# A gated scan with two feed-forward layers: first loads in halves on two queues, turns set among products, output weights loaded by rows

## The reference

```
f = lower_bound + (1 - lower_bound) * sigmoid(f_logit)
h[t] = f[t] * h[t-1] + (1 - f[t]) * x[t]              (per batch and channel)
z = relu(h @ w_in1) ** 2 @ w_out1
g = z @ w_in2 ;  out = where(g > 0, g, exp(min(g, 0)) - 1) @ w_out2
```

## Time and profile before

| | us |
|---|---|
| median of 3 runs | 1981.14 (1980.86 to 1981.81) |
| profiled execution, its own time | 1982.25 |
| its span | 1980.5 |
| PE busy | 1968.4 |
| DVE busy | 1575.6 |
| ACT busy | 1510.4 |
| POOL busy | 608.8 |

### The profile page before, as it was taken

One profiled execution on the slowest core, in us unless ns is written; L12 is line 12 of the kernel. 1 busy time (PEld: TensorE's weight loads), 2 busy tenths in 40 slices (PEclk: granted clock), 3 DMA queues, 4 the chain that ended last, 5 costly groups with the idle time before them and its releaser, 6 DMA issues.

```text
span 1980.5 us, 27947 instructions
## 1 busy us (share of the span) xinstructions
PE 1968.4 (99%) x8746; PEld 1638.7 (83%) x8746; DVE 1575.6 (80%) x1766; ACT 1510.4 (76%) x1818; POOL 608.8 (31%) x506
## 2 busy tenths in 40 slices
PE   8999999999999999999999999999999999999998
PEld 6887888888888888888888888888888888888888
DVE  5656888888888888888888888878888887866887
ACT  7887778778778777777877777777777787777766
POOL 3455323223232232332323323223232232322410
PEclk9999999999999999999999999999999999999999
DMA  5679444444444444344444444434444443443453
GB/s 168 198 210 266 152 139 121 147 146 132 131 137 137 123 146 146 115 146 137 126 135 146 135 134 135 138 107 156 146 125 143 137 124 116 147 128 121 139 171 111
DMA packets 244291, 283.09 MB, mean 143 GB/s; under 512 B 170433, under 2 KB 180674, under 8 KB 244162
## 3 DMA queue, kind: packets, MB, share of 16 engines
q1 hardware_dynamic: 241250, 280.23, 46.6%
q10 hardware_dynamic: 2912, 1.51, 0.3%
HBM read 249.30 MB, written 32.37 MB: 142 GB/s over the span
## 4 chain that ended last, share of the span: by engine, by line
PE 97%; ACT 1%; DMA 1%; issue 0%; SPq 0%; DVE 0%; ACTq 0%
PE acc L586 51%; PE ring L586 45%; DMA o_sb<-in_moe_w_in_dram 0%; PE acc L739 0%; DMA xa<-in_f_logit_dram 0%; PE ring L729 0%; ACT xa L985 0%; ACT xa L980 0%; ACT xb L980 0%; SPq L404 0%; ACT xb L985 0%; ACT hid_hi L1043 0%; ACT hid_hi L1053 0%; ACT wout L919 0%; DVE y_raw L1442 0%
## 5 line engine op out<-in xcount | busy, mean ns | idle before, releaser
L586 PE MATMUL acc<-hid_hi,wout 128*128 128x512 f32 (+1 forms) x3072 | 1142.4, 387 | 1.4 <-DVE wout L1277 1.3
L586 PE MATMUL ring<-t_hi,s_w 128*128 128x512 f32 (+1 forms) x2720 | 1035.7, 387 | 2.5 <-ACT m_sb L1064 1.4
L586 PEld LDWEIGHTS acc<-hid_hi,wout 128*128 128x128 f32 x3072 | 576.6, 188 | 115.7 <-DVE hid_lo L1361 2.2
L586 PEld LDWEIGHTS ring<-t_hi,s_w 128*128 128x128 f32 x2720 | 510.6, 188 | 104.9 <-ACT m_sb L1064 1.8
L586 PE MATMUL acc<-hid_lo,wout 128*128 128x512 f32 (+1 forms) x1536 | 594.7, 387 | 0.0
L586 PE MATMUL ring<-t_lo,s_w 128*128 128x512 f32 (+1 forms) x1360 | 526.6, 387 | 0.0
L1690 POOL TENSOR_TENSOR xb<-xb,m_sb 128x512 f32<-128x512 f32 (+1 forms) x176 | 225.9, 1284 | 965.4 <-DVE hid_lo L1361 960.8
L1064 ACT ACTIVATE m_sb<-ring 128x512 f32<-128x512 f32 (+1 forms) x176 | 104.6, 594 | 365.2 <-PE ring L586 345.7
L586 PEld LDWEIGHTS acc<-hid_lo,wout 128*128 128x128 f32 x1536 | 288.3, 188 | 56.5
L586 PEld LDWEIGHTS ring<-t_lo,s_w 128*128 128x128 f32 x1360 | 255.3, 188 | 50.6
L1361 DVE TENSOR_TENSOR hid_lo<-xa,hid_hi 128x1024 fp32r<-128x1024 f32 (+1 forms) x191 | 231.4, 1211 | 80.6 <-ACT hid_hi L1043 80.5
(11 more groups left out here) (117 smaller groups left out, 1711.9 us busy)
## 6 DMA issues: line engine op xcount, KB each, us to landing
s_w<-s_kept SPq DMA_DIRECT2D x184, 512.0 KB, 3.8
s_w<-s_kept SPq DMA_DIRECT2D x176, 384.0 KB, 4.1
wout<-w_kept SPq DMA_DIRECT2D x96, 512.0 KB, 4.4
out_dram<-o_sb SPq DMA_DIRECT2D x88, 128.0 KB, 3.5
f_raw<-in_f_logit_dram SPq DMA_DIRECT2D x168, 64.0 KB, 3.5
x_raw<-in_x_dram SPq DMA_DIRECT2D x168, 64.0 KB, 2.7
s_kept<-ee SPq DMA_DIRECT2D x16, 512.0 KB, 3.8
s_kept<-s_w SPq DMA_DIRECT2D x8, 512.0 KB, 3.9
```

The lines of the kernel that those rows point to most:

```text
L586: mm = nc.tensor.matmul(out_ap, lhs[a], rhs[b], start=start and t == 0, stop=stop and t == 2)
```

## The change

- `load_first` loads half of a 512 KB tile, 256 KB. The halves of f of batch 1 are the first issue on SP and on ACT, then come the halves of x of batch 1. f of batch 0 is also split over the two queues; x of batch 0 goes out as two halves on SP, behind the first two pairs' raw weights. The row of `lower_bound` moves from SP to ACT.
- `turn` takes one chunk. PE's order is f chunk 0, `lower_bound`, f chunk 1, x of batch 1, 4 matmuls on zeros in place of 16, f chunk 0 of batch 0; the other three turns stand between the first products.
- ACT makes the gates of batch 0 ahead of the cast of batch 1's second chunk, and `weights_hi_out(1, 0)` stands before the first relu. DVE's order follows.
- The second layer's output weights are loaded with one DMA of whole rows for a pair; ACT and DVE put the columns in order, with two instructions of 128x256 each in place of one of 128x512.
- In the phase of order 1, SP issues the next pair's raw loads before the stores, the quarters of f and x in steps 1, 4 and 5 at the end in place of 1, 4 and 6 near the start, and `load_s` before `load_sums`. `load_s` of the first pairs has a wait of its own.
- The last quarter's `tanh` of block 2 and the last pair's `weights_hi_out`/`weights_lo_out` of layer 2 move from the end of order 1 into step 0 of order 2, behind the copies of m1 and m2. `keep_w2` of that pair moves behind the first `load_w2`.

```diff
-WARM = (8, 16)
+WARM = (8, 4)
...
+        def load_first(eng, src, b, dst, loaded, half):
+            o = dst[:, b, half].rearrange("p (k d) -> p k d", d=D)
+            rows = src[b, half * HALF:(half + 1) * HALF, :].rearrange("(k p) d -> p k d", p=P)
+            eng.dma_start(o, rows).then_inc(loaded[b], DMA_INC)
...
+        def columns_in(t, c):
+            return t.rearrange("p j (a c e) -> p c j a e", c=CH, a=G)[:, c]
+        def columns_new(t, c):
+            return t[:, :, c * P:(c + 1) * P].rearrange("p j (a e) -> p j a e", a=G)
...
-        W_LOADS = {1: DMA_INC, 2: 2 * CH * DMA_INC}
+        W_LOADS = {1: DMA_INC, 2: DMA_INC}
...
     (load_raw_out, second layer)
-                for j in range(2):
-                    for c in range(CH):
-                        sp.dma_start(o[:, j, c * P:(c + 1) * P].rearrange("p (a e) -> p a e", e=SQ),
-                                     wout2_v[:, 2 * p + j, :, c, :]).then_inc(wr_loaded[0], DMA_INC)
+                sp.dma_start(o, wout2_v[:, 2 * p:2 * p + 2, :]).then_inc(wr_loaded[0], DMA_INC)
...
     (load_s)
-                if not (isinstance(pr.s, int) and pr.s < 2):
+                if isinstance(pr.s, int) and pr.s < 2:
+                    sp.wait_ge(up_n0, pr.g - 1)
+                else:
                     sp.wait_ge(m4_done, pr.s - 1)
...
+            QUARTER_AT = {1: 1, 4: 2, 5: 3}
...
     (SP's phase, order 1)
                         if p < PAIRS - 1:
                             load_q(ahead(p + 1))
                         else:
+                            load_s(ahead(p + 1))
                             load_sums(ahead(p + 1))
-                            load_s(ahead(p + 1))
-                        if p in (1, 4, 6):
-                            load_f(2, (p + 1) // 2)
-                            load_x(2, (p + 1) // 2)
+                        if 1 <= p < PAIRS - 1:
+                            load_raw_in(2, p + 1)
+                        load_raw_out(2, p)
                         if p >= 1:
                             keep_w2(p - 1)
-                        load_raw_out(2, p)
                         keep_q(2, p)
                         if p == 0:
                             keep_sums(1, PAIRS - 1)
                         else:
                             keep_sums(2, p - 1)
-                            if p < PAIRS - 1:
-                                load_raw_in(2, p + 1)
+                        if p in QUARTER_AT:
+                            load_f(2, QUARTER_AT[p])
+                            load_x(2, QUARTER_AT[p])
                         continue
                     if known(ph.order, 2) and p == 0:
+                        load_s(ahead(1))
                         load_sums(ahead(1))
-                        load_s(ahead(1))
                     if known(ph.order, 2) and p == 0:
                         keep_sums(2, PAIRS - 1)
-                        keep_w2(PAIRS - 1)
...
                     if ph.layer == 2:
                         sp.wait_ge(down_n0, g - 1)
                         load_w2(pair_of(ph, p))
-            load_first(sp, f_logit, 1, xa, f0_loaded)
-            sp.dma_start(lb_row, lower_bound.rearrange("(o d) -> o d", o=1)).then_inc(lb_loaded, DMA_INC)
+                    if known(ph.order, 2) and p == 0:
+                        keep_w2(PAIRS - 1)
+            load_first(sp, f_logit, 1, xa, f0_loaded, 0)
+            load_first(sp, x, 1, xb, x0_loaded, 0)
             load_raw_in(1, 0)
+            load_first(sp, f_logit, 0, xa, f0_loaded, 0)
             load_raw_in(1, 1)
-            load_first(sp, x, 0, xb, x0_loaded)
+            for h in range(2):
+                load_first(sp, x, 0, xb, x0_loaded, h)
             load_raw_out(1, 0)
...
     (PE; turn(b, c, ...) now turns one chunk c and waits for both halves of its load)
-            turn(1, xa, f_turn, f0_loaded, None, f0_turned)
+            turn(1, 0, xa, f_turn, f0_loaded, None, f0_turned)
             pe.wait_ge(lb_loaded, DMA_INC)
...
-            turn(1, xb, x_turn, x0_loaded, None, x0_turned)
+            turn(1, 1, xa, f_turn, f0_loaded, None, f0_turned)
+            for c in range(CH):
+                turn(1, c, xb, x_turn, x0_loaded, None, x0_turned)
             warm(WARM[1])
+            turn(0, 0, xa, f_turn, f0_loaded, tanh0_done, f0_turned)
             pe.wait_ge(y0_lo, 1)
             up_ready(pr0, 1)
             up_half(pr0, 1, 0)
-            turn(0, xa, f_turn, f0_loaded, tanh0_done, f0_turned)
+            turn(0, 1, xa, f_turn, f0_loaded, tanh0_done, f0_turned)
+            turn(0, 0, xb, x_turn, x0_loaded, x0_gated, x0_turned)
             pe.wait_ge(consts_done, 2)
             up_ready(pr1, 1)
             up_half(pr1, 1, 0)
-            turn(0, xb, x_turn, x0_loaded, x0_gated, x0_turned)
+            turn(0, 1, xb, x_turn, x0_loaded, x0_gated, x0_turned)
             pe.wait_ge(y0_lo, 2)
...
     (ACT, weights_hi_out; the same in DVE's weights_lo_out with a subtraction)
+                for c in range(CH):
+                    w = nc.scalar.activation(columns_new(o, c), columns_in(w_slot(layer, p), c), ACT.Copy)
+                w.then_inc(w_hi, 1)
...
     (ACT, hosted)
-                    if at == (7, "d"):
+                    if at == (7, "d") and not ph.plain():
                         tanh(ph.i + 1, 3)
+                if known(ph.order, 2):
+                    if at == (0, "c"):
+                        tanh(2, 3)
+                    if at == (0, "d"):
+                        weights_hi_out(2, PAIRS - 1)
...
-                    if place == "d":
+                    if place == "d" and p < PAIRS - 1:
                         weights_hi_out(2, p)
...
-            load_first(act, x, 1, xb, x0_loaded)
-            load_first(act, f_logit, 0, xa, f0_loaded)
+            load_first(act, f_logit, 1, xa, f0_loaded, 1)
+            act.dma_start(lb_row, lower_bound.rearrange("(o d) -> o d", o=1)).then_inc(lb_loaded, DMA_INC)
+            load_first(act, x, 1, xb, x0_loaded, 1)
+            load_first(act, f_logit, 0, xa, f0_loaded, 1)
...
             quarters_hi(1, 1)
+            gates0(0)
             split0(1, 1)
-            gates0(0)
+            weights_hi_out(1, 0)
...
             plain_square(pr1, 1)
             hi_of_n1(pr1)
-            weights_hi_out(1, 0)
             plain_act(pr0, 0)
...
     (DVE, hosted, and its opening)
-                    if place == "c":
+                    if place == "c" and p < PAIRS - 1:
                         weights_lo_out(2, p)
+                if known(ph.order, 2) and at == (0, "c"):
+                    weights_lo_out(2, PAIRS - 1)
...
             scan0(1, 1)
+            gate0(0, 0)
             lo0(1, 1)
-            gate0(0, 0)
             scan0(0, 0)
             gate0(0, 1)
             lo0(0, 0)
             scan0(0, 1)
+            weights_lo_out(1, 0)
             lo0(0, 1)
...
-            weights_lo_out(1, 0)
             quarters_lo(1, 2)
```

More of the change, by code:

```diff
@@ L261, in gated_scan_two_ffn @@
         x_turn = acc[:, 0]
-        def load_first(eng, src, b, dst, loaded):
-            o = dst[:, b].rearrange("p n s -> p (n s)").rearrange("p (k d) -> p k d", d=D)
-            eng.dma_start(o, src[b, 0:S, :].rearrange("(k p) d -> p k d", p=P)).then_inc(loaded[b], DMA_INC)
+        def load_first(eng, src, b, dst, loaded, half):
+            o = dst[:, b, half].rearrange("p (k d) -> p k d", d=D)
+            rows = src[b, half * HALF:(half + 1) * HALF, :].rearrange("(k p) d -> p k d", p=P)
+            eng.dma_start(o, rows).then_inc(loaded[b], DMA_INC)
         def r_place(layer, p):
@@ L348, in _ @@
             wout1_v = w_out1.rearrange("(j p) d -> p j d", p=P)
-            wout2_v = w_out2.rearrange("(j p) (a c e) -> p j a c e", p=P, a=G, c=CH)
+            wout2_v = w_out2.rearrange("(j p) d -> p j d", p=P)
             def load_rows(src, b, t0, n, dst, loaded, parts=range(G)):
@@ L729, in warm, with turn @@
                     nc.tensor.matmul(ring[:, t % 2, :], zeros[:, 0:P], zeros[:, 0:BANK], start=True, stop=True)
-            def turn(b, src, dst, loaded, read, turned):
+            def turn(b, c, src, dst, loaded, read, turned):
                 rows = src[:, b].rearrange("p n s -> p (n s)").rearrange("p (k e c) -> p k c e", e=P, c=CH)
[L734 to L740, removed]
+                pe.wait_ge(loaded[b], 2 * DMA_INC)
+                if b == 0:
+                    pe.wait_ge(read, c + 1)
+                for k in range(S // P):
+                    mm = nc.tensor.transpose(dst[:, c, k * P:(k + 1) * P], rows[:, k, c], ident)
+                mm.then_inc(turned, 1)
             pr0, pr1 = pair_of(first(0), 0), pair_of(first(0), 1)
@@ L918, in weights_hi_out @@
                     o = wout2[:, p % 2, :, 0, :]
-                nc.scalar.activation(o, w_slot(layer, p), ACT.Copy).then_inc(w_hi, 1)
+                if layer == 1:
+                    nc.scalar.activation(o, w_slot(layer, p), ACT.Copy).then_inc(w_hi, 1)
+                    return
```

(13 more changed lines are left out.)

## The result

The changed kernel takes 1976.24 us (median of 10 runs, 1976.04 to 1977.13) against 1981.2 (10 runs, 1980.42 to 1981.9): 5.0 us less, ratio 0.9975 with a 95% interval of 0.9966 to 0.9985. The forecast was 1976.5. The profiled execution took 1976.04, its span is 1974.3: 6.2 less than the profiled execution before. The two gains differ because the execution profiled before was 1.05 us slower than its kernel's median and this one 0.2 faster. In 80 executions beside the experiments the kernel before took from 1979.39 to 1983.9, and a single execution of it can stand some 2 us off its median.

A forecast was written before the change was run, and what follows sets the result against it. PE, busy nearly throughout, bounds the kernel, so only an earlier start of its unbroken stretch or closed gaps help. Opening 3.1 plus change of phase 1.5 gives 4.6 us off the median 1981.14: 1976.5 us, range 1974.9 to 1979.0.

The forecast's parts named there:

- (a): Opening, first load: f ahead of x on both queues, so PE's first turn starts at 5.2, 1.3 us earlier.
- (b): Opening, first turn to end of first low part: the 6.88 us stay as they were.
- (c): Opening, to the first product: four warm-up matmuls for sixteen no longer hold PE past the low part, 1.4 us earlier.
- (d): Opening, first product to relu of n1: 0.55 us fewer turns on PE, 0.45 given back waiting for the second low part.
- (e): Opening, relu of n1 to relu of n0: moving the output weights' cast to where ACT waits gains 0.5 us.
- (f): Opening, relu of n0 to the end of DVE's subtraction: 4.83 us of casts, untouched.
- the change of phase: Last plain phase to first seven-product phase: PE's waits for m1 and s_w go, 1.5 us, between 0.2 and 1.55.
- The wait of 0.45 for the second low part: Opening, between first products: PE ready at 16.55, second low part at 17.0 because it now follows batch 0's gates.
- rival 4: Opening: clock rises earlier, during x's turns, saving 0.4 to 0.8 us more; total gain 5.0 to 5.4, 1975.9; chance 0.18.
- rival 1: First load: splitting brings nothing, the turn still starts at 6.57, 1.3 us lost, total gain 3.3, 1977.8; chance 0.12.
- Rival 3: Opening: with fewer warm-ups the low clock lasts through it, matmuls at 0.43; 3.2 us slower, 1984.3; chance 0.05.
- both waits: Change of phase: PE's waits of 0.2 us for s_w and 1.36 for ACT's copy of m1, both to go.

## Why the prediction was right

By its own steps, expected and measured gain in the profile (us):

| step | expected | measured |
|---|---|---|
| (a) the first load | 1.3 | 1.45 |
| (b) first turn to first low part | 0 | 0.84 |
| (c) warm-up | 1.4 | 1.36 |
| (d) between products | -0.07 | -0.13 |
| (e) the weights' cast | 0.5 | 0.51 |
| (f) the last casts | 0 | 0 |
| the change of phase | 1.5 | 2.11 |

The wait of 0.45 for the second low part is as worked out.

- The load: right, and for the stated reason. On one queue, undivided, the turn starts at the same 5.12. Eleven profiles with f in halves at the head of both queues have it between 4.99 and 5.71, the two with x beside f at 6.53 and 6.57. The rule of the Trainium skill (DMA: Bandwidth & Descriptors, Rules for kernel authors), that halves (there by partition) and a second queue bring no bandwidth, agrees with these rows. It does not say that f must then land as late as before, and rival 1 falls: x no longer stands beside it.
- The clock: the mechanism of rival 4, given 0.18, is what happened, beside the forecast's own. f's second four turns took 0.74 us in ten of the thirteen profiles of changed kernels and 1.12 to 1.13 in the other three. Those three need 6.85 to 6.86 us from turn to low part, with the same turns in the same order, and the ten 5.71 to 6.57; so at the slow pitch the new order gives 0.03, and the 0.84 came with the clock. (What the fast pitch would give with the old order, in which ACT's first scale waited 0.91 us for the constants, no run shows.) So (b) is the term of the opening that was mis-sized. I took the stretch of 6.88 from a trace in which all of it ran at the slow pitch. An early rise need not last: in two of the ten (the first loads and the change of phase as before) the granted clock fell to 0.50 again while PE was turning. PE had waited 1.66 and 0.94 us for f shortly before. It is 0.50 from 9 to 12 us in the first and from 8 to 10 us in the second.
- Rival 3 did not happen in the changed kernel, but the profiled execution of the kernel with the turns in twos shows its mechanism, products at 0.43, over six matmuls.
- The change of phase: both waits went as forecast. Undoing the move of tanh and casts brings PE's wait for m1 back; undoing the row loads brings back the one for s_w. The size was not right: 2.11 in place of 1.5. I took the idle time as the price. From the start of the down product ahead of m5 to m5 (188.73 to 190.93) it was 2.20 us where 0.68 is usual, so 1.52 lost and 0.14 more in the next matmuls for 1.36 of idle; and across the wait for s_w, 0.19 idle, the lead of the changed kernel grows from 4.00 to 4.48. The waits put back by the experiments cost alike, 1.78 for 1.5 and 1.88 for 1.6. So a wait of PE costs its idle time and about 0.3 us more, of which 0.16 is how idle time is counted: a matmul's modelled 0.39 us reaches 0.16 past the start that the next would have had.
- What hid the two low terms, 1.4 us together, in the comparison of medians: the profiled execution before stood 1.05 above its median and the one after 0.2 below. Part of what the first lost must be lost in some runs only; a late clock is the likely part, but the kernel before has one profile, and at which pitch it usually turns stays open. The parts undone one by one (1.8, 0.6, 0.5, 0.7 and 1.9 us of medians, with the 0.5 that the late s_w cost before) sum to 6.0, also above the 5.0 of the medians.

So the median was met within 0.3 us by a sum whose parts were right in kind and, against the profiles, 1.5 too low. That the total fits is luck: the 1.5 us that the terms lacked were nearly made up by the 1.25 us by which the two profiled executions stand off their medians.

## What to carry to other kernels

When one engine is busy throughout, look only for what its unbroken stretch waits for at its start, follow that as one chain of stretches, and price a mid-stream wait at its idle time and about 0.3 us more, as measured here. Put the load that the chain begins with alone at the head of a queue; splitting it is not needed. Put small turns in the engine's waits: moving one there gave 1.0 us. When a load comes late, look first at when its queue issued it, and only then at how long it took. And compare a profiled execution with the median of its kernel before terms are taken from it.

## What the runs showed that I had not expected

- Kernels whose first turns are the same ran them at either pitch (the first four from 0.71 to 1.10 us), so one profiled execution of a short opening can be some 0.8 us off.
- The two DMA queues did not share alike: 0.96 MB on ACT's against 0.48 on SP's from 4 to 8 us before.
- From the end of the opening on, eight of the eleven changed kernels whose change of phase was free of waits agree to 0.02 us over 1928.5. The two with the casts in a new order took 0.08 more and the one with SP's order as before 0.19.
